# First attention of a three-part kernel: V stationary, P divided on GpSimd, keys loaded in bands

## The reference

```python
# 1. banded attention, B=2, H=8, S=768, D=64
scores = scale * q @ k.T                    # keep: key < n_global, or 0 <= row - key < n_local
scores = where(keep, scores - slope[h] * dist, -1e9)
a = exp(scores - max(scores)); a = a / (sum(a) + 1e-9)
x = a @ v                                   # -> (B, S, 512)
# 2. MoE of four causal attention experts (wq, wk, wv, wo), two of four by gate
# 3. u = x + (U V along the sequence); out = u + relu(u @ w_ch1) @ w_ch2
```

## Time and profile before

| | |
|---|---|
| median of 3 runs | 522.91 us (521.49 to 524.48) |
| profiled execution, its own time | 521.91 us |
| its span, first to last instruction | 520.1 us |
| TensorE busy | 483.1 us, 93% |
| VectorE / ScalarE / GpSimd busy | 228.5 / 187.6 / 80.2 us |
| mean granted TensorE clock | 0.98 |
| first attention | scores start at 8.3 us, `project(0)` starts at 118.4 us |

### The profile page before, as it was taken

One profiled execution on the slowest core, in us unless ns is written; L12 is line 12 of the kernel. 1 busy time (PEld: TensorE's weight loads), 2 busy tenths in 40 slices (PEclk: granted clock), 3 DMA queues, 4 the chain that ended last, 5 costly groups with the idle time before them and its releaser, 6 DMA issues.

```text
span 520.1 us, 8734 instructions
## 1 busy us (share of the span) xinstructions
PE 483.1 (93%) x3368; PEld 420.2 (81%) x3368; DVE 228.5 (44%) x710; ACT 187.6 (36%) x485; POOL 80.2 (15%) x57
## 2 busy tenths in 40 slices
PE   2999999989996888978799999999999999999997
PEld 1888888869984776857589988888888788888886
DVE  3477766643479658375815512222222212222212
ACT  1676777733044557456833311111111211111112
POOL 0023300000005200050025201111122101111110
PEclk9999999988998999979999999999999999999999
DMA  6946333002015020130021101111111113211103
GB/s 224 288 120 202 113 113 113 1 1 62 1 27 164 33 61 2 32 112 1 2 82 42 39 23 41 42 42 40 42 42 41 42 38 84 81 62 42 40 1 121
DMA packets 20842, 34.54 MB, mean 66 GB/s; under 512 B 5216, under 2 KB 8160, under 8 KB 20800
## 3 DMA queue, kind: packets, MB, share of 16 engines
q1 hardware_dynamic: 20800, 33.97, 21.9%
HBM read 27.67 MB, written 3.15 MB: 59 GB/s over the span
## 4 chain that ended last, share of the span: by engine, by line
PE 84%; DVE 8%; ACT 3%; issue 3%; DMA 1%; SPq 0%; DVEq 0%; ACTq 0%
PE ps_s L985 25%; PE ps_o L985 16%; PE ps_t L985 13%; PE ps_o L1038 7%; PE ps_t L1019 5%; PE ps_o L1162 3%; PE ps_s L1005 3%; PE ps_t L1146 3%; DVE prob L655 3%; PE ps_s L1130 2%; PE ps_s L1004 2%; ACT prob L460 1%; PE ps_s L1002 1%; PE ps_o L1046 1%; ACT probT L517 1%
## 5 line engine op out<-in xcount | busy, mean ns | idle before, releaser
L610 ACT ACTIVATE hidh<-ps_o 128x768 fp32r<-128x768 f32 x32 | 26.0, 812 | 181.4 <-PE ps_o L985 181.4
L460 ACT ACTIVATE prob<-prob,smin 128x256 f32<-128x256 f32 (+3 forms) x144 | 77.2, 543 | 28.0 <-DVE smin L655 28.0
L968 DVE SCALAR_TENSOR_TENSOR hidl<-ps_o,hidh 128x768 fp32r<-128x768 f32 x32 | 30.6, 958 | 95.0 <-ACT hidh L610 95.0
L419 POOL TENSOR_TENSOR fl<-fraw,fh 128x512 fp32r<-128x512 f32 x32 | 41.3, 1291 | 177.6 <-DVE fh L897 177.6
L985 PE MATMUL ps_s<-hidh,fl 128*128 128x512 f32 x128 | 50.5, 394 | 0.0
L985 PE MATMUL ps_s<-hidl,fh 128*128 128x512 f32 x128 | 50.2, 392 | 0.0
L985 PE MATMUL ps_s<-hidh,fh 128*128 128x512 f32 x128 | 50.1, 391 | 0.0
L897 DVE CAST fh<-fraw 128x512 fp32r<-128x512 f32 x32 | 13.6, 426 | 71.5 <-PE ps_t L985 71.5
L985 PE MATMUL ps_o<-xl,w01h 128*128 128x256 f32 (+1 forms) x128 | 43.3, 338 | 0.0
L985 PE MATMUL ps_o<-xh,w01h 128*128 128x256 f32 (+1 forms) x128 | 43.2, 338 | 0.0
L985 PE MATMUL ps_o<-xh,w01l 128*128 128x256 f32 (+1 forms) x128 | 43.1, 337 | 0.0
(11 more groups left out here) (175 smaller groups left out, 1096.1 us busy)
## 6 DMA issues: line engine op xcount, KB each, us to landing
fraw<-in_w SPq DMA_DIRECT2D x32, 256.0 KB, 2.6
wraw<-in_w SPq DMA_DIRECT2D x8, 512.0 KB, 3.7
qT<-in_q SPq DMA_DIRECT2D x8, 384.0 KB, 3.2
kT<-in_k SPq DMA_DIRECT2D x8, 384.0 KB, 3.8
vN<-in_v SPq DMA_DIRECT2D x8, 384.0 KB, 4.8
out<-prob SPq DMA_DIRECT2D x12, 256.0 KB, 2.6
vB<-in_v SPq DMA_DIRECT2D x8, 192.0 KB, 5.0
mkh<-mkh SPq DMA_DIRECT2D x8, 192.0 KB, 2.6
```

The lines of the kernel that those rows point to most:

```text
L419: return pool.tensor_tensor(lo, raw, hi.bitcast(F32), ALU.subtract)
L460: act.activation(prob_s, prob_s, ACT.Exp, bias=smin[:, col:col + 1], scale=-1.0, accum_out=ssum[:, col:col + 1]).then_inc(done, 1)
L610: act.activation(hidh[:, f % 2, :], ps_o[:, 0:S], ACT.Relu).then_inc(hidh_done, 1)
L968: dve.scalar_tensor_tensor(hidl[:, f % 2, :], ps_o[:, 0:S], 0.0, hidh[:, f % 2, :].bitcast(F32), ALU.max, ALU.subtract).then_inc(hidl_done, 1)
```

## The change

V becomes the stationary operand of the values product, 64 columns for each head, and the two heads write to the two halves of the PSUM partitions; the output is x transposed already. Since a column of P^T is then a row of the output, the division moves ahead of the product: GpSimd multiplies P by the inverse of its sum. K is loaded as one 256-key band for each tile, so that a score product is one matmul; the first 32 keys of the bands are copied on chip by GpSimd. The stages are spread further (values three duos behind, x four). Evacuations are shared between ScalarE and VectorE, and ScalarE makes the hi part of x.

```diff
+ACT_EVACS = N_UNIT // 4
+QK_IN = 16 * NT
+def by_act(u):
+    return u % 4 == 0
+        a_prob = [... for n in range(12)]
+        a_score = [ps_s[:, 2 * d + par, 2 * P * e:2 * P * (e + 1)] for d in range(2) for e in range(2) for par in range(2)]
@@ sync: load_pair
-                sp.dma_start(kT[:, p % 2, :], t["k"][b, pr]).then_inc(qk_in[p], 16)
+                sp.dma_start(kT[:, p % 2, 0:2 * P], t["k"][b, pr, :, 0:2 * P]).then_inc(qk_in[p], 16)
+                for i in range(2, NT):
+                    sp.dma_start(kT[:, p % 2, 2 * P * (i - 1) + FIRST:2 * P * i],
+                                 t["k"][b, pr, :, P * (i - 1) + FIRST:P * (i + 1)]).then_inc(qk_in[p], 16)
@@ sync: order of the loads
                 load_pair(2)
                 load_weights(1)
+                load_pair(3)
                 load_weights(2)
-                load_pair(3)
                 load_weights(3)
                 for p in range(4, B * HP):
                     load_pair(p)
@@ gpsimd (weight_lo(n): half of a weight's rest, after wh_done n // 2 + 1; wl_done after each second)
+            def first(p):
+                slot = kT[:, p % 2, :].rearrange("p (i n) -> p i n", i=NT - 1)
+                pool.wait_ge(qk_in[p], QK_IN)
+                pool.tensor_copy(slot[:, 1:NT - 1, 0:FIRST],
+                                 slot[:, 0:1, 0:FIRST].broadcast_to([P, NT - 2, FIRST])).then_inc(first_keys, 1)
+            def safe(d):
+                four = slice(4 * d, 4 * d + 4)
+                pool.wait_ge(exp_done, 4 * d + 4)
+                pool.tensor_scalar(seps[:, four], ssum[:, four], EPS, None, ALU.add).then_inc(safe_done, 1)
+            def divide(d):
+                pool.wait_ge(inv_done, d + 1)
+                for s in range(4 * d, 4 * d + 4):
+                    a, z = band_cols(s // 2 % NT)
+                    x = a_prob[s % 12][:, 0:z - a]
+                    pool.tensor_scalar(x, x, sinv[:, s:s + 1], None, ALU.mult).then_inc(norm_done, 1)
+                first(0)
+                for d in range(N_DUO + 1):
+                    if d % X_PARTS == 0 and d // X_PARTS + 1 < B * HP:
+                        first(d // X_PARTS + 1)
+                    if 1 <= d <= N_DUO:
+                        safe(d - 1)
+                        divide(d - 1)
+                    if 5 <= d < 5 + 8:
+                        weight_lo(d - 5)
@@ scalar
+            def x_hi(d):
+                p, n = divmod(d, X_PARTS)
+                act.wait_ge(pv_done, d + 1)
+                act.activation(xh[:, p // HP, p % HP, 2 * n * P:2 * (n + 1) * P],
+                               ps_o[:, 512 * (d % 2):512 * (d % 2) + 2 * P], ACT.Copy).then_inc(xh_done, 1)
+                for d in range(N_DUO + 4):
+                    if 3 <= d < N_DUO + 3 and by_act(2 * (d - 3)):
+                        evac(2 * (d - 3))
                     if d < N_DUO:
                         for s in range(4 * d, 4 * d + 4):
                             a, z = band_cols(s // 2 % NT)
+                            exp_step(s, a_prob[s % 12][:, 0:z - a], s, (sub_done, s + 1), exp_done)
+                    if d >= 4:
+                        x_hi(d - 4)
@@ vector (evac(u): tensor_copy of ps_t to a_probT after t_done; x_lo(d): xl = ps_o - xh after xh_done)
             def attend(s):
-                dve.wait_ge(s_done, s + 1)
+                dve.wait_ge(s_done, (s | 2) + 1)
             def inverse(d):
-                dve.wait_ge(exp_done, 4 * d + 4)
-                dve.tensor_scalar(seps[:, four], ssum[:, four], EPS, None, ALU.add).then_inc(inv_done, 1)
+                dve.wait_ge(safe_done, d + 1)
                 dve.reciprocal(sinv[:, four], seps[:, four]).then_inc(inv_done, 1)
                 for d in range(N_DUO + 4):
-                    if d >= 4:
-                        x_out(d - 4)
                     if 3 <= d < N_DUO + 3:
-                        scale_out(d - 3)
+                        for u in (2 * (d - 3), 2 * (d - 3) + 1):
+                            if not by_act(u):
+                                evac(u)
                     if d < N_DUO:
+                        attend(4 * d)
+                        attend(4 * d + 1)
                     if 1 <= d <= N_DUO:
                         inverse(d - 1)
+                    if d < N_DUO:
+                        attend(4 * d + 2)
+                        attend(4 * d + 3)
+                    if d >= 4:
+                        x_lo(d - 4)
@@ tensor
             def scores(u):
+                if i == 2:
+                    pe.wait_ge(first_keys, p + 1)
+                    if s >= 8 and u % 2 == 0:
+                        pe.wait_ge(sub_done, s - 8 + 3)
+                    keys = slice(0, P) if i == 0 else slice(2 * P * (i - 1), 2 * P * i)
+                    pe.matmul(a_score[s % 8][:, 0:keys.stop - keys.start], qT[half, p % 2, i * P:(i + 1) * P],
+                              kT[half, p % 2, keys], start=True, stop=True, skip_group_check=True).then_inc(s_done, 1)
             def transposes(u):
-                    pe.wait_ge(exp_done, s + 1)
+                    pe.wait_ge(norm_done, s + 1)
             def values(d):
+                            last = pe.matmul(ps_o[half, at:at + P], v, a_probT[u % 4][:, par, n * P:(n + 1) * P],
+                                             start=n == 0, stop=own, skip_group_check=True)
-            def x_turn(d):
                 for d in range(N_DUO + 3):
                     if d < N_DUO:
                         scores(2 * d)
                         scores(2 * d + 1)
-                    if 1 <= d <= N_DUO:
-                        transposes(2 * d - 2)
-                        transposes(2 * d - 1)
+                    if d >= 3:
+                        values(d - 3)
                     if 2 <= d < N_DUO + 2:
-                        values(d - 2)
-                    if d >= 3:
-                        x_turn(d - 3)
+                        transposes(2 * d - 4)
+                        transposes(2 * d - 3)
```

More of the change, by code:

```diff
@@ L122, in build @@
         hidl = sb("hidl", [P, 2, S], F32R)
-        a_prob = [prob[:, n // 2, 384 * (n % 2):384 * (n % 2) + 2 * P] for n in range(8)]
+        a_prob = [prob[:, n // 3, 2 * P * (n % 3):2 * P * (n % 3 + 1)] for n in range(12)]
+        a_score = [ps_s[:, 2 * d + par, 2 * P * e:2 * P * (e + 1)] for d in range(2) for e in range(2) for par in range(2)]
         a_probT = [probT[:, n // 2, n % 2, 0:4 * P].rearrange("p (a n) -> p a n", a=2) for n in range(4)]
@@ L167, in build @@
         rel = sb("rel", [P, S], where=att)
-        kpos = sb("kpos", [P, S], where=att)
-        dist = sb("dist", [P, S], where=att)
+        kpos = sb("kpos", [P, 3 * P], where=att)
+        dist = sb("dist", [P, 3 * P], where=att)
         near = sb("near", [P, S], where=att)
@@ L244, in build @@
         dist_step, bias_done = sem("dist_step"), sem("bias_done")
-        s_done, sub_done, exp_done, inv_done, norm_done, t_done, evac_done, pv_done, xt_done, xh_done, xl_done = (
-            sem("a_" + n) for n in ("s", "sub", "exp", "inv", "norm", "t", "evac", "pv", "xt", "xh", "xl"))
+        first_keys, safe_done, inv_done, norm_done = (sem("a_" + n) for n in ("first", "safe", "inv", "norm"))
+        s_done, sub_done, exp_done, t_done, evac_act, evac_dve, pv_done, xh_done, xl_done = (
+            sem("a_" + n) for n in ("s", "sub", "exp", "t", "evac_act", "evac_dve", "pv", "xh", "xl"))
         wh_done, wl_done, w_proj = sem("wh_done"), sem("wl_done"), sem("w_proj")
@@ L429, in _, with weight_lo @@
-            pool.wait_ge(wh_done, 4)
             ro = wraw[:, 1, 0:EP * DM].rearrange("p (c n) -> p c n", c=EP)
-            lo_of(ro, wo_h[:, :, :], wo_l[:, :, :]).then_inc(wl_done, 1)
+            def weight_lo(n):
+                k, half = divmod(n, 2)
+                raw, hi, lo = [(r[0], wqk_h[:, :, 0:256], wqk_l[:, :, 0:256]),
+                               (r[1], wqk_h[:, :, 256:512], wqk_l[:, :, 256:512]),
+                               (rv, wv_h[:, :, :], wv_l[:, :, :]), (ro, wo_h[:, :, :], wo_l[:, :, :])][k]
+                rows = slice(half * raw.shape[1] // 2, (half + 1) * raw.shape[1] // 2)
+                pool.wait_ge(wh_done, k + 1)
+                done = lo_of(raw[:, rows, :], hi[:, rows, :], lo[:, rows, :])
+                if half:
+                    done.then_inc(wl_done, 1)
@@ L433, in _ @@
+            with pool.Else():
+                for n in range(8):
+                    weight_lo(n)
             pool.wait_ge(wh_done, 5)
@@ L755, in _ @@
                             dve.wait_ge(bias_done, 2 * (d // X_PARTS + 1))
-                        for s in range(4 * d, 4 * d + 4):
-                            attend(s)
+                        attend(4 * d)
+                        attend(4 * d + 1)
                     if 1 <= d <= N_DUO:
                         inverse(d - 1)
+                    if d < N_DUO:
[3 more added lines that the diff above has]
+                        x_lo(d - 4)
```

(29 more changed lines are left out.)

86 lines of the change are left out of this document (33 added, 53 removed).

## The result

The change makes the kernel slower: 546.73 us median (543.79 to 548.69, 4 runs) against 522.91, a ratio of 1.045 [1.039, 1.051]. Forecast were 534 and a range of 518 to 546, so the sign was right and the size too small. The profiled execution took 545.64 us, span 543.7.

The account below looks back on a forecast made before the run. The loop was to end on the handover between VectorE and ScalarE instead of TensorE. Terms +1.9, +0.9, +5.8, +1.8, +2, +1.3 and -2.8 make +10.9 us: median 522.9 becomes 534, range 518 to 546.

Parts of the forecast that it names:

- term 3: Keys of pair 4, queued behind load_weights(3), arrive late and hold GpSimd's iteration 9 and VectorE's reciprocal: +5.8 us.
- term 2: 18 VectorE iterations from iteration 6, with roundings of weights now on the path: 73.8 us against 72.9, +0.9.
- The new loop on VectorE: x_lo waits for ScalarE's x_hi behind four exps: VectorE idle 1.3 us, iterations of 3.94 us on average against 4.05.
- TensorE's relief arrives: Rival: x_lo's wait is short and iterations take 3.1 us, 17 us less over 18: 519 us; chance 15%.
- GpSimd is the bound: Rival: GpSimd's divisions set the loop; 538 us at 0.75 us a division, 550 at 1.0; chance 15%.
- Term 1: Start up to VectorE's iteration 6: GpSimd's copy waits for pair 2's keys, iteration 6 starts at 36.5: +1.9 us.
- the keys are in time: Rival: loads of keys are not late, so terms 1, 3, 4 and 6 vanish: 523 us; chance 12%.
- Term 4: Keys of pairs 3, 5, 6 and 7 come 0.3 to 1.2 us late each: +1.8 us.
- Term 6: TensorE's clock falls to the lower level for some 7 us after an idle 5 in iteration 9: +1.3 us.
- the clock stays low: Rival: TensorE idles a microsecond each iteration and a third of the loop runs at 1.2 GHz: 545 us; chance 8%.
- Term 5: Port shared by VectorE and GpSimd: roundings or biases meet divide or weight_lo in five iterations, 0.4 us each: +2 us.
- Term 7: Tail from iteration 24 to part 2, without x_turn and a last VectorE round trip and with a denser TensorE: -2.8 us.

Follow-up runs that it names:

- e12: The changed kernel with pair 4's keys loaded before the weights, x_hi before the exps, two-input division and later copy of first keys, without filling products: 507.5 us.
- e14: The changed kernel with two edits, the division as a two-input product and the copy of first keys behind the division, one iteration later: 524.0 us.
- e16: e12 with x_hi written back behind the four exponentials: 17.1 us more than e12.
- e15: e12 with the division written back as in the changed kernel, one value per partition: 533.1 us.
- e13: The changed kernel with one edit, the copy of first keys behind the division, one iteration later: 12.9 us less than the changed kernel.
- e2: The changed kernel with GpSimd dividing only the first two columns of each P, every wait and instruction kept: 546.9 us.
- e3: The changed kernel with only SyncE's queue reordered, pair 4's load ahead of load_weights(3): 5.7 us less by medians, not clear of noise.
- e9: The changed kernel with one edit, the division as a two-input product with the reciprocal repeated along the row: ratio 1.034, about 541 us.
- e6: e2 with two more unused TensorE products of 256 columns in each duo, filling its pauses: 534.9 us.
- e1: The changed kernel with GpSimd multiplying P by constant 1.0 instead of the inverse row sum: a difference of 3.1 us, not clear of noise.

## Why the prediction was right in its direction and wrong in its size

The prediction's own way of counting, from VectorE's iteration 6 and its iteration 24 to part 2, can be read off the changed kernel:

```profile
38.03 1.01 DVE L735 COPY probT<-ps_t 128x256 f32<-128x256 f32 x2
...
134.11 1.01 DVE L735 COPY probT<-ps_t 128x256 f32<-128x256 f32 x2
```

Iteration 6 starts 3.4 us later than before (1.9 forecast), the 18 iterations take 96.1 us for 72.9, 23.2 more (11.8 forecast, terms 2 to 6), and the tail takes 8.8 for 10.9, 2.0 less (2.8 forecast). Together that is 24.55 for 10.9; the loop holds 11.4 of the 13.7 us that were missed. Two sums in the working are slightly off, without weight: by its own rates 1.5 MB take 3.8 us, not 4.0 (term 3), and four roundings at 0.6 and two biases at the 0.33 of the old trace are 3.1, not 2.7 (term 2).

- **What leaves TensorE: right.** The sixteen values instructions take about 1.1 us and the duo's TensorE work stays near 3.1: e12's whole iteration is 3.07. The relief is real, and with the change as written none of it arrives.
- **The new loop on VectorE: right to a hundredth.** x_lo at S+2.84 for S+2.85, idle 1.31 for 1.3, and where GpSimd, keys and clock are out of the way (e14, 68 to 108 us) an iteration of 3.96 for 3.94. e16 against e12 prices the handover at 17.1 us, which is what the rival "TensorE's relief arrives" gave for its absence (17), with its 3.1 us for an iteration. In the changed kernel itself the handover isn't what ends last: GpSimd comes after it.
- **Term 2 (18 iterations): failed.** It counted 4.1 us for a full iteration, 3.94 on average; GpSimd sets 4.2 even where no load is late, and 5.0 to 5.9 where half a weight comes behind the divisions. The step that failed is the price of the division in the part "GpSimd": 0.45 us taken, by likeness to the cast, the bound 0.75, and 0.95 measured. Four are 3.63 us for 1.8. The likeness was chosen on the number of tensors read, and by the rows that is not what sets this price: the form that takes the reciprocal as a second tensor is the cheaper one. Alone among otherwise cured kernels it costs 25.6 us (e15), with the handover in place 9.8 (e13 to e14), in the presence of the copy next to nothing (e2). The rival "GpSimd is the bound" had this mechanism, and for 1.0 us its 550 us; 546.7 lies between its two times.
- **Term 1 (up to iteration 6).** The copy of pair 2's keys ended its wait at 25.81 where 25 was forecast, as described. Iteration 6 started at 38.03, for 36.5. The term left out pair 1's keys, whose copy waited 6.5 us in iteration 0 (1.3 of them counted), and the dear divisions. TensorE's pause, 3.15 us before 29.19, was as forecast.
- **Term 3 (keys of pair 4): mechanism and way of the load right, the loss too small.** From the issue of q at 58.13 to the copy at 64.38 are 6.25 us, forecast 6.1. VectorE lost 8.69 us, for 5.8: GpSimd was itself already late at that point. e3, which undoes the order of the loads, gives back 5.7.
- **Terms 3, 4 and 6 together: mis-sized.** Terms 1, 3, 4 and 6 were 10.8 us. The late copy, which takes the keys out of the divisions' way, measured 12.9 us behind a dear division and 19.6 behind a cheap one. The second rival, "the keys are in time", said 523 for a kernel with the handover and a hidden division; e14 measured 524.0. That is luck in part: e14 reached iteration 6 at 30.77, 3.9 us earlier than the old loop, took 77.5 us for the 18 iterations where 75.8 are forecast without keys and clock, and had a tail of 11.4, with the clock at 0.50 over 112 to 116, for 8.1. What it does show is that the excess over it lies in division and keys.
- **Term 4.** 0.3 to 1.2 us late each was forecast for pairs 3, 5, 6 and 7; in the changed kernel only pair 7's copy waited, 0.98, because GpSimd itself was late. A faster GpSimd only reaches them sooner: the copies' waits (the start's 7.7 among them) were 24.5 us in the changed kernel, 34.2 in e9, 41.0 in e2. What the prediction left out is that this wait grows where another is cured. Together with the clock (e6) this is why e2 gained nothing; for e1 and e9, which gained little, the rows fit the same account.
- **Term 6 (clock): mis-sized.** +1.3 for one fall, at pair 4. The clock fell there as foreseen, and also before it (0.58 over 28 to 32) and after it (0.59 over 80 to 84, 0.57 over 100 to 104): 0.86 over 121 us. In the kernel with two columns divided filling the pauses is worth 12.0 us (e2 against e6); in the changed kernel itself it gave 2.5. The rival "the clock stays low", by pauses of one microsecond in a duo, is not what happened: e14 has those pauses and holds 1.00 from 68 to 108 us. Longer pauses stand before the falls, those for keys and, as e13 shows, those of 2.3 to 3.1 us in a loop whose keys are in time. Not every long one does it: in the changed kernel 2.57 us before 91.11 were followed by 1.00.
- **Term 5 (the shared port): about right, on GpSimd's side.** Four divisions of one iteration with a bias and a cast of VectorE in them, against four of the same sizes without:

```profile
31.05 3.54 POOL L470 TENSOR_SCALAR prob<-prob,sinv 128x128 f32<-128x128 f32 x4 [0.31 <-DVE sinv L742]
...
115.30 2.98 POOL L470 TENSOR_SCALAR prob<-prob,sinv 128x128 f32<-128x128 f32 x4 [0.30 <-DVE sinv L742]
```

```profile
33.38 0.96 DVE L779 CAST wqk_h<-wraw 128x1024 fp32r<-128x1024 f32 x1
```

The division that started at 33.11, ahead of that cast, took 1476 ns for 923, and the cast 0.96 for 0.69. Over the eight groups of four that meet a bias or a cast, GpSimd loses 2.5 us in all, 0.1 to 0.6 each; the term said 2, and it falls on the engine that sets the loop. The lock that the prediction cites, whole and for whoever starts first, is not what these rows show: the division that started first was lengthened, and by more than the cast. A copy out of PSUM that started at 121.90, inside four divisions of GpSimd, took 0.68 us, as long as before. The case that stood open in the prediction, copies of VectorE locked out too for 16 us, did not come about; the Trainium skill, SBUF — State Buffer, section Who interferes with whom, had them left alone, and the trace agrees. The casts of the first two weights took 917 ns on average, for 687 before, the third 0.78 us, and that of the fourth 684 ns.
- **Term 7 (tail): nearly right, 2.0 us less for 2.8.** Part 2's first product now takes 0.48 us for 0.78, as expected of the full clock; the tail as a whole took 8.8 us, where its steps add up to 8.9 and 0.8 more were taken off for the clock.

By e13 and e14 the excess of 22.7 us over e14 divides into 12.9 for the copy and 9.8 for the division, in that order of removal. In the other order the division gets about 1% and the copy 3.2% (e9, by ratios). The parts aren't additive, so no single split is the true one; that both had to go is shown. e6, which met the sum's 534 with 534.9, did so with other parts than the sum's: its copies still waited 39.0 us.

## What to carry to other kernels

Before a short instruction with a wait of its own is put at the head of an in-order queue, ask what stands behind it and doesn't need it: here seven copies of 0.3 us, one iteration too early, cost 10 to 20 us. When removing a suspect changes nothing, that doesn't clear it; look which wait grew by what was won, and remove both. Price an elementwise instruction on GpSimd by a row of the same instruction, and take a bound from its cousins only if it is wide. When a total meets its forecast, compare the parts as well: e6 and e14 met theirs with other parts.

## What the runs showed of the hardware that wasn't expected

On GpSimd the product with one value per partition is dearer than that of two tensors. For 256 and 128 fp32 columns it took 953 and 613 ns (875 and 546 with a constant), against 615 to 642 and 399 to 402 ns for the two-input product with the value repeated along the row. For two columns it took 294 ns. The Trainium skill, GPSIMD Engine Reference, section 4.1 Engine selection, has GpSimd at about line rate with one input and about twice as slow as VectorE with two; of these two forms the rows have the second as the quicker one, and the measurement decides.

A wait for a load can cost TensorE more than its length: after 8.19 us without work it ran at 0.50 over 68 to 72 us. Filling all pauses was worth 12.0 us in e6 against e2. Pauses of 0.5 to 1.5 us in each duo went with a clock of 1.00 (e14, 68 to 108 us); behind most of those of 2.3 to 3.1 us it fell (e13).

A VectorE cast of 0.7 us lengthened a GpSimd division that had started before it by 0.55 us, and took 0.27 us longer itself (33.11 and 33.38 in the changed kernel).
